# First two chunks of an mLSTM: exponents built on TensorE from the gate rows, and stabilizers, weights and states moved behind their outputs

## What is computed

```
for t in range(S):                       # every batch and head
    m_new  = max(f[t] + m, i[t])
    C = exp(f[t] + m - m_new) * C + exp(i[t] - m_new) * outer(v[t], k[t])
    n = exp(f[t] + m - m_new) * n + exp(i[t] - m_new) * k[t];  m = m_new
    y[t] = sigmoid(o[t]) * (C @ q[t]) / max(|n . q[t]|, 1)
x = y as (1536, 320);  h = x @ w_in      # 320 -> 2048
x = (h - tanh(h)) @ w_out                # 2048 -> 320
out = sum over 4 experts e of p[:, e] * (relu(x @ w1[e]) @ w2[e])   # 320 -> 1024 -> 320
```

## Time and profile before

| | |
|---|---|
| median of three runs | 649.0 us (648.75 to 649.26) |
| the profiled execution's own time | 649.84 us |
| its span in the trace | 648.0 us |
| TensorE (PE) busy | 96% of the span |
| DVE, ACT, POOL busy | 43%, 29%, 16% |
| first product of the layer-1 loop | at 42.75 us |
| mean DMA rate | 50 GB/s |

### The profile page before, as it was taken

How to read it: one execution, slowest core, us unless ns; L and a number is a source line. 1 busy time by engine, 2 the same in 40 slices (tenths; PEclk the granted TensorE clock), 3 DMA queues, 4 the chain that set the end, 5 groups by cost and what they waited for, 6 DMA issues and landing times.

```text
span 648.0 us, 8940 instructions
## 1 busy us (share of the span) xinstructions
PE 621.7 (96%) x3728; PEld 554.8 (86%) x3728; DVE 277.0 (43%) x504; ACT 185.7 (29%) x329; POOL 105.1 (16%) x87
## 2 busy tenths in 40 slices
PE   3997989999999999998999999999999999999998
PEld 2777988999878788887999999999999999999997
DVE  5576677776666465544131322313131331313132
ACT  2424534323442425455111232111321111111111
POOL 2356530000000000656000152000430000000000
PEclk8579799999999999999999999999999999999999
DMA  7254242112100000233100022000200000001011
GB/s 266 76 170 150 95 151 67 63 64 65 65 1 2 0 1 1 90 123 102 45 2 1 0 90 91 1 0 1 73 17 1 1 1 0 1 1 41 2 41 40
DMA packets 9831, 32.42 MB, mean 50 GB/s; under 512 B 1502, under 2 KB 3646, under 8 KB 9790
## 3 DMA queue, kind: packets, MB, share of 16 engines
q0 software_dynamic: 3456, 17.30, 7.8%
q1 hardware_dynamic: 6334, 14.54, 6.7%
HBM read 29.68 MB, written 1.97 MB: 49 GB/s over the span
## 4 chain that ended last, share of the span: by engine, by line
PE 84%; DVE 9%; ACT 3%; issue 2%; DMA 1%; SPq 0%; DVEq 0%; ACTq 0%
PE bank L858 9%; PE bank L859 9%; PE bank L860 9%; PE bank L900 9%; PE bank L901 9%; PE bank L902 9%; PE bank L862 5%; PE bank L861 5%; PE bank L877 3%; PE bank L762 3%; PE bank L878 3%; PE bank L879 3%; PE bank L753 2%; DVE g_lo L709 2%; DVE g_tmp L701 2%
## 5 line engine op out<-in xcount | busy, mean ns | idle before, releaser
L722 DVE SCALAR_TENSOR_TENSOR g_lo<-bank,g_hi 128x512 fp32r<-128x512 f32 x96 | 66.4, 692 | 256.3 <-ACT g_hi L514 256.2
L514 ACT ACTIVATE g_hi<-bank 128x512 fp32r<-128x512 f32 x96 | 57.5, 599 | 272.5 <-PE bank L862 272.4
L900 PE MATMUL bank<-w_all,g_hi 128*128 128x320 f32 x384 | 118.3, 308 | 1.5 <-DVE x_hi L679 1.5
L858 PE MATMUL bank<-x_hi,w_all 128*128 128x512 f32 (+2 forms) x320 | 118.9, 371 | 0.6 <-DVE x_hi L638 0.6
L859 PE MATMUL bank<-x_lo,w_all 128*128 128x512 f32 (+2 forms) x320 | 118.5, 370 | 0.0
L860 PE MATMUL bank<-x_hi,w_all 128*128 128x512 f32 (+2 forms) x320 | 118.3, 370 | 0.0
L901 PE MATMUL bank<-w_all,g_hi 128*128 128x320 f32 x384 | 118.3, 308 | 0.0
L902 PE MATMUL bank<-w_all,g_lo 128*128 128x320 f32 x384 | 118.2, 308 | 0.0
L386 POOL TENSOR_TENSOR w_all<-w_raw,w_all 128x1408 fp32r<-128x1408 f32 x16 | 51.4, 3211 | 238.6 <-ACT w_all L435 238.6
L900 PEld LDWEIGHTS bank<-w_all,g_hi 128*128 128x128 f32 x384 | 72.1, 188 | 5.5 <-issue 1.9
L901 PEld LDWEIGHTS bank<-w_all,g_hi 128*128 128x128 f32 x384 | 72.1, 188 | 4.5
(11 more groups left out here) (119 smaller groups left out, 741.2 us busy)
## 6 DMA issues: line engine op xcount, KB each, us to landing
w_raw<-in_w POOLq DMA_DIRECT2D x24, 704.0 KB, 4.4
feat<-in_feat SPq DMA_DIRECT2D x12, 512.0 KB, 4.1
tok<-in_tok SPq DMA_DIRECT2D x12, 484.0 KB, 5.6
out<-arena SPq DMA_DIRECT2D x12, 160.0 KB, 1.9
gst<-split SPq DMA_DIRECT2D x24, 4.0 KB
zx<-split SPq DMA_DIRECT2D x24, 4.0 KB
g_tmp<-in_gates SPq DMA_DIRECT2D x2, 48.0 KB
probs<-in_probs SPq DMA_DIRECT2D x1, 24.0 KB, 1.9
```

What stands on the lines that cost most here:

```text
L514: A(g_hi[:, b, 0:N], h_ps[b][:, 0:N], ACT.Relu).then_inc(ghi_ready, 1)
L722: V.scalar_tensor_tensor(g_lo[:, b, 0:N], h_ps[b][:, 0:N], 0.0, g_hi[:, b, 0:N].bitcast(F32), ALU.max, ALU.subtract).then_inc(g_ready, 1)
L858: mm(h, up_part(m, 0, k), x_hi[:, k, c], start=k == 0, stop=False)
L900: mm(out, g_hi[:, b, t], high_w, start=first, stop=False)
```

## The change

It has five parts. (1) Chunks 0 and 1 get their exponents without `gst` and `zx`: `first_exponents` multiplies `g_high` and `g_low` by columns of an identity `ident_r` spread over 512 columns, and for each head and each part of e one product of 128 columns with a broadcast identity column; then the mask. (2) The order on DVE is: gate rows, gate of chunk 0, scores of chunks 0 and 1, their rows (`first_rows`, read straight from the sums in PSUM), `x_low(0)`, then the stabilizers, `x_low(1)`, and the operand `zx`. The fillings of `gst`, `zx` and `state` go to POOL. (3) Weights (`wa`) and the states of chunks 0 and 1 stand inside the loop, at m = 0 and m = 1. (4) `START` of chunks 2 to 10 goes up by 4, 3, 2, 2, 2, 2, 1, 1 and 1; chunk 2 is wholly in the loop. Pieces 1 and 2 of the weights are split at the end of steps 0 and 1, and on POOL `split_low(0)` stands ahead of `weigh_v(0)`. (5) ACT's queue issues two of the three gate loads; SP's queue orders its loads as feat, tok of chunk 0, then of chunk 1, then of chunk 2 once tok of chunk 0 has landed, and its stacks begin with chunk 2.

```diff
-START = {2: -2, 3: 3, 4: 8, 5: 13, 6: 17, 7: 21, 8: 26, 9: 31, 10: 36, 11: 42}
+START = {2: 2, 3: 6, 4: 10, 5: 15, 6: 19, 7: 23, 8: 27, 9: 32, 10: 37, 11: 42}
-WARM_UP = 8
-FILL = 4
+WARM_UP = 3
-        split_at = {0: -1, 1: -1, 2: -1}
+        split_at = {0: -1, 1: 0, 2: 1}
...
+            for n in range(2):
+                load_feat(n)
+                load_tok(n)
+            sp.wait_ge(tok_in[0], 16)
+            load_feat(2)
+            load_tok(2)
+            sp.dma_start(probs[:, :, :], probs_d).then_inc(probs_in, 16)
...
+            stack(2)
+            stack(3)
             for n in range(RING, STEPS):
-                sp.wait_ge(e_ready, 2 * n - 2)
-                stack(n, z_high, z_low)
                 sp.wait_ge(sums_ready, n - RING + 1)
                 load_feat(n)
                 sp.wait_ge(y_ready, n - RING + 1)
                 load_tok(n)
+                if n + 1 < STEPS:
+                    sp.wait_ge(e_ready, 2 * n)
+                    stack(n + 1)
...
+            def first_rows(n, o_ps):
+                dve.wait_ge(intra_ready, n + 1)
+                after(dve, y_ready, n)
+                sums = heads(o_ps[:, 0:HEADS * HDE])
+                rows_out(n, sums[:, :, 0:HD], sums[:, :, HD:HDE].rearrange("p h a -> p (h a)"))
...
+            sigmoid(0)
             scores(0, 0, up_ps[0])
             scores(0, 1, up_ps[1])
-            sigmoid(0)
             scores(1, 0, bank[0])
             scores(1, 1, bank[1])
-            first_sums(0, c_ps, bank[4])
-            finish_rows(0)
+            first_rows(0, c_ps)
             sigmoid(1)
-            first_sums(1, up_ps[0], up_ps[1])
-            finish_rows(1)
+            first_rows(1, up_ps[0])
             x_low(0, c_ps)
+            stabilizers()
             x_low(1, up_ps[0])
...
+            def first_exponents(n, banks):
+                r = row0(n)
+                for q, out in enumerate(banks):
+                    picked = ident_r[:, r + q:r + HEADS:2]
+                    for k, rows in enumerate((g_high, g_low)):
+                        mm(out[:, :], rows, spread(picked, CH), start=k == 0, stop=False)
+                    for j in range(QUAD):
+                        row = r + 2 * j + q
+                        for rows in (e_high, e_low):
+                            mm(out[:, j * CH:(j + 1) * CH], ident_r[:, row:row + 1].to_broadcast([ROWS, P]), rows,
+                               start=False, stop=False)
+                    mm(out[:, :], ident_b[:, :], mask[:, :, :], start=False, stop=True).then_inc(e_ready, 1)
...
             for m in range(ALL_STEPS):
                 up(m)
+                if m == 0:
+                    weigh_columns()
+                if m == 1:
+                    new_state(0, a_ps, 0)
+                    new_state(1, b_ps, 0)
                 for n, k in phase(m):
                     attention(n, k)
```

More of the change, by code:

```diff
@@ L458, in _ @@
             A(e_high, er, ACT.Copy).then_inc(ehi_done, 1)
+            gate(0)
+            exps(0, 0, bank[0])
+            exps(0, 1, bank[1])
+            gate(1)
+            exps(1, 0, a_ps)
+            exps(1, 1, b_ps)
+            split_high(0)
+            x_high(0, c_ps)
+            x_high(1, up_ps[0])
             act.wait_ge(z_rows, 1)
@@ L465, in _ @@
             A(beta[:, :], decay[:, 0:ROWS], ACT.Exp).then_inc(beta_ready, 1)
[L466 to L481, removed]
             def evac(g):
@@ L516, in _ @@
                     evac(m // L1_TILES - 1)
-                for k in range(RING, PIECES):
+                for k in range(1, PIECES):
                     if split_at[k] == m:
@@ new lines, in rows_out @@
+            def rows_out(n, sums, nq):
+                chain.done(V.tensor_scalar(dn[:, :], nq, -1.0, None, ALU.mult))
+                chain.wait()
+                chain.done(V.scalar_tensor_tensor(dn[:, :], nq, 1.0, dn[:, :], ALU.max, ALU.max))
+                chain.wait()
+                chain.done(V.reciprocal(dn[:, :], dn[:, :]))
+                chain.wait()
+                o = tok[:, n % RING, 2 * D + HEADS:3 * D + HEADS].rearrange("p (h d) -> p h d", d=HD)
+                y = num[:, :, 0:HD]
+                chain.done(V.tensor_tensor(y, sums, spread(dn[:, :], HD), ALU.mult))
+                chain.wait()
+                after(dve, t_ready, n - 1)
+                V.tensor_tensor(yt[:, n % 2, :].rearrange("p (h d) -> p h d", d=HD), y, o, ALU.mult).then_inc(y_ready, 1)
@@ L794, in _ @@
                 mm(bank[7][:, 0:P], ident[:, :], ident[:, :], start=True, stop=True)
+            pe.wait_ge(identb_ready, 1)
+            pe.wait_ge(mask_ready, 1)
+            keep_warm(7, bank[7])
+            pe.wait_ge(identr_ready, 1)
+            pe.wait_ge(ghi_done, 1)
+            pe.wait_ge(glo_done, 1)
+            pe.wait_ge(ehi_done, 1)
+            pe.wait_ge(elo_done, 1)
+            first_exponents(0, bank[0:2])
+            scores(0, up_ps[0:2])
+            first_exponents(1, (a_ps, b_ps))
@@ L795, in _ @@
+            pe.wait_ge(exp_done, 2)
+            scores(1, bank[0:2])
+            keep_warm(3, bank[4])
+            intra(0, c_ps)
+            keep_warm(3, bank[4])
+            intra(1, up_ps[0])
             pe.wait_ge(top_ready, 1)
             for k, src in enumerate((top, cum)):
-                last = nc.tensor.transpose(c_ps[:, k * P:k * P + ROWS], src[:, CH - 1:CH].to_broadcast([ROWS, P]),
+                last = nc.tensor.transpose(bank[4][:, k * P:k * P + ROWS], src[:, CH - 1:CH].to_broadcast([ROWS, P]),
@@ L809, in _ @@
-            last.then_inc(weigh_t, 1)
-            pe.wait_ge(exp_done, 2)
-            scores(1, bank[0:2])
-            intra(0, c_ps)
-            pe.wait_ge(wa_ready, 1)
-            new_state(0, bank[4], 0)
-            pe.wait_ge(exp_done, 4)
-            both_exponents(2, (a_ps, b_ps))
-            intra(1, up_ps[0])
-            new_state(1, up_ps[1], 0)
-            pe.wait_ge(exp_done, 6)
-            scores(2, (a_ps, b_ps))
-            keep_warm(FILL, bank[0])
+            keep_warm(4, bank[3])
@@ L822, in _, with weigh_columns @@
             turn(0, c_ps)
-            keep_warm(FILL, bank[0])
+            keep_warm(8, bank[3])
             turn(1, up_ps[0])
-            keep_warm(FILL, bank[0])
+            keep_warm(6, bank[3])
+            def weigh_columns():
+                pe.wait_ge(weigh_done, 2)
+                pe.wait_ge(decay_ready, 1)
+                for k in range(2):
+                    last = nc.tensor.transpose(bank[4][:, k * ROWS:(k + 1) * ROWS], weigh[:, k, :],
+                                               ident[0:ROWS, 0:ROWS])
+                last.then_inc(weigh_t, 1)
```

149 lines of the change are left out of this document (61 added, 88 removed).

## The result

| | before | changed |
|---|---|---|
| median of four runs | 648.88 us (648.23 to 649.26) | 664.17 us (662.19 to 666.35) |
| the profiled execution's own time | 649.84 us | 666.35 us |
| its span | 648.0 us | 664.6 us |
| first product of the layer-1 loop | 42.75 us | 43.38 us |
| last product of up(16), start | 104.82 us | 111.87 us |

The ratio of the changed kernel to the one before is 1.0238, with a 95% interval of 1.0204 to 1.0271. The forecast was 648.0 us with a range of 642 to 652.5; the time lies outside it. Two of the ten runs of `a_gates_sp` (662.3 and 663.0 us) and, the other way, one of the six of `k_after_start9` (649.67 us) took some 12 us more or less than the rest of their kernel; none of the three has a trace, and the ratios compare the rest.

What follows compares the result with a forecast made beforehand. TensorE, busy 96% of the span, gains only where it waits or runs slowly: loop start 29.1 + 17.4 + 57.3 = 103.8 us to up(16) against 104.8, 1 us off the 649.0 median gives 648.0 us, range 642 to 652.5.

Steps and rivals of the forecast that it cites:

- Part 1, the clock: Ahead of the loop: clock rises about 1 us into the exponents, 0.4 us lost, bounds 0 and 6.4 us.
- The fifth rival: Half clock all the way ahead of the loop: loop starts at 40 us, time 659 us; chance 0.06.
- Part 1, the gates: At the start: two queues may bring gates up to 0.7 us sooner; counted as nothing, bounds 0 and 0.7 us.
- until about 7.1 us: Ahead of the exponents: seven keep_warm products at half clock, 0.43 us each, hold TensorE until then.
- Part 2: Steps 0 to 3: ACT waits for piece 3, so scores of chunk 2 start 17.4 us after the loop's start.
- Part 3: From the scores of chunk 2 to the last product of up(16): 57.3 us, against 46.8 us before.
- two more steps: Scores of chunk 2 to up(16): changed kernel has two extra steps, 1.95 us each with gaps, 3.9 us added.
- the comparison point: Start of the last product of up(16): 104.82 us before, forecast 103.8 us, 1 us faster.
- the later START: Behind up(16): START one or two steps later for chunks 5 to 10, counted 0, bound 0.5 us slower.
- 3.2 us by the prediction's count: Work moved into the loop: exponents and scores of chunk 2, states, weights; 3.2 us.

Runs made afterwards that it cites:

- a_gates_sp: Changed kernel with all three gate loads issued first on SP's queue, ahead of feat and tok, none by ACT: 650.92 us, ratio 1.0026.
- k_after_start9: Changed kernel with START of chunks 9 and 10 put back to 31 and 36, from 32 and 37: median 660.85 us.
- h_gates_warm2: Changed kernel with all gate loads first on SP's queue and 2 instead of 7 keep_warm products ahead of the exponents: 662.87 us, ratio 1.0216.
- b_warm14: Changed kernel with 14 instead of 7 keep_warm products ahead of the first exponents, gates still late: 651.62 us, ratio 1.0050.
- f_start9_back: Changed kernel with gates on SP, 9 keep_warm products, piece 3 split one step later, START of chunks 9 and 10 back: 648.6 us, ratio 0.9979.
- i_low_after_rows: Kernel before with first_exponents for chunks 0 and 1, 9 keep_warm, and POOL's low parts held until the rows stand: 640.37 us, ratio 0.9854.
- j_low_and_fill: As i_low_after_rows, with eight instead of four unread wide products ahead of each of the two transposes of rows: 640.19 us, ratio 0.9859.
- e_before_filled: Kernel before with 28 more keep_warm products while TensorE waited for zx: 646.9 us, ratio 0.9965.

## Why the prediction was wrong

**Part 1, the clock, failed, and with it the forecast.** The text took "a rise about 1 us into the exponents (0.4 us lost)" with "bounds 0 and the full 6.4 us". In the changed kernel the clock rose at 41 us, 30 us after the exponents had begun. The bound was too narrow as well, since it let only the exponents be slow: scores, fillings and intra behind them were slow too. The reason given was that TensorE runs wide products "without a gap" from about 4 us on. There was a gap of 2.37 us ahead of the exponents. `h_gates_warm2` and `b_warm14` show from both sides that the clock decides: same gates with less filling 662.87 us, late gates with more filling 651.62. From the first exponents to the loop's start it took 33.0 us where the sum had 22.0, so this term was off by 11.0 us: 12.1 by the clock (`a_gates_sp` takes 20.9 us for the same stretch, 7.33 to 28.26), less 1.1 by which the sum was too long. The fifth rival named this outcome with a loop start at 40 us and 659 us, and gave it 0.06.

**Part 1, the gates, failed.** They were counted at "0 and 0.7 us" earlier and came 3 us later; the exponents began at 10.38 instead of 7.1 us, off by 3.3 us. Two of three gate loads stand on ACT's queue, the last asked for at 2.44 us, and had to share the engines with the loads of feat and tok that SP asked for from 1.75 us on; the last gate landed 5.55 us after its issue. In the kernel before the last was asked for no earlier, at 2.60 us, but ahead of feat and tok, and DVE used it at 5.03. With all three ahead of feat and tok on SP's queue the scan starts at 4.96 us. The Trainium skill, "DMA: Bandwidth & Descriptors", section "Issuing engines are not separate DMA queues", also says that transfers interleave on the same engines whoever starts them. The trace agrees; I had used only its half on issue time, and not asked what interleaves with the gates. The gap behind the filling comes from this delay, so the two failures are one chain. The filling itself came later too, at 4.84 us against 3.72 in `a_gates_sp`: ACT makes `ident_b`, for which it waits, only after it has issued the two loads. The prediction had it run "until about 7.1 us"; it ended at 8.01. That the filling would have been too short even with the gates in time is ruled out by `a_gates_sp`, which reached its loop at 28.26 us against the 29.1 that I had forecast for the changed kernel.

**Part 2 was right.** 18.35 us measured, 17.4 forecast, by the same chain and with the same wait on ACT. The load of piece 3 took 6.8 us to ACT's start where I had 5.5.

**Part 3 was 2.8 us too long.** From the scores of chunk 2 to up(16) it took 50.1 us; the scores and sums of chunk 5, which my 57.3 included and which now stand behind up(16), add 4.3, so 54.5 us. Of the 2.8 us, 1.95 are a step too many: the sum took "two more steps", but the scores of chunk 2 stand at step 3 in the changed kernel and those of chunk 3 at step 4 before, which is one more. The windows confirm half clock in 61.7 to 68 us, 6.3 us at 0.51 and so about 3.1 us lost, where I had kept 3.4.

**Behind the comparison point the later START was counted at "0 (bound 0.5 us slower)"; 5.2 us were lost there.** From up(16) to the end it is 552.7 us, of which 4.3 are the work of chunk 5 named above, against 543.2 before. I had seen that the rows of chunk 8 come at step 31, and not that the exps of chunk 9 then meet the evaluation of group 2's inputs at step 32. `k_after_start9` gives 3.6 us back; where the other 1.6 are lost is not shown.

**The terms add up.** 14.3 (gates 3.3, clock 11.0) + 0.95 - 2.8 + 5.2 = 17.6 us; the forecast span was 647.0, the measured one 664.6, that of the slowest of the four runs.

**Where did the 14 us of the early start go in `a_gates_sp`?** The structure of the forecast holds there: its loop is 14.5 us earlier and its time the same as before. Part 2's wait on ACT is in its trace too (8.07 us before L435 at 42.74), and the scores of chunk 2 start 18.15 us after the loop. That its traced span is 647.0 us, the very number of the forecast, is in part luck: with the 4.3 us of chunk 5 it is 2.1 us ahead of the forecast at up(16) (97.42 us), and the same 2.1 us are lost behind it, where the forecast had 0; its median is 650.92. The rest is lost at steps 0 to 16, seen best between two kernels without the loss at step 34. From the loop's start to up(16), with the sums of chunk 5 in it, `f_start9_back` takes 72.5 us (28.32 to 96.46, and 4.3), `i_low_after_rows` 64.0 (30.33 to 94.36), and the kernel before 62.1. The work that the change moves into the loop is 3.2 us by the prediction's count. The other 5 us are waits and half clock: from its loop's start to 60 us TensorE is idle for 6.7 us at a mean clock of 0.78 in `f_start9_back`, and for 4.1 us at 0.84 in `i_low_after_rows`. So the new exponents were the gain, and moving weights, states and chunk 2 behind the loop's start, which was to clear the way to it, gave back more than the 2 us of earlier start that it brought over `i_low_after_rows`. How much each of these moves gave back alone is not separated.

## What to carry to other kernels

When a forecast rests on the clock, look for the idle time directly ahead of the dense work and at what ends it. Filling products must reach up to that work, sized by the latest plausible arrival of what it waits for; too many cost nothing that could be measured (`b_warm14`, `j_low_and_fill`), too few cost 12 us here. And small transfers that everything waits for belong in front of the large ones in time of issue; a second issuing engine did not put them there.

## What the runs showed of the hardware

- One filling of seven wide products, followed by idle times of 0.41, 1.69 and 2.37 us, left the exponents at full clock, at full clock for one bank and then at half, and at half from the start. In the changed kernel TensorE then worked from 10.4 to 41 us nearly without idle time at the durations of half clock, on products of 512, 128 and 41 columns; what it did just before the rise was eight `keep_warm` products between two sets of transposes; in the kernel before it was four.
- The Trainium skill, "TensorE: Matmul & The Clock Gate", section "HAM oscillation — how this bites in real kernels", describes work that begins at the low clock after each wait; its waits are of 3 to 5 us. The traces agree for the waits of 2.37 and 2.83 us ahead of the exponents and in part for that of 1.69 us (the second bank), not for those of 0.41, 0.69 and 1.43 us (`e_before_filled`). In the loop the same wait goes both ways: behind 1.50 us ahead of the sums of chunk 3 the clock fell in `i_low_after_rows` (0.52 from 54 to 60 us) and stayed at 1.00 in `j_low_and_fill`. Nor does a fall need a wait: ahead of the loop of `i_low_after_rows` the clock was at half from about 23.5 to 27 us, and TensorE had not been idle for more than 0.22 us at a time since 8 us. What decides between such cases is not shown here.

```profile
23.00:24.00 1.00, 1.00 (x17) 0.78 (x14) 0.97 (x2) 0.00 (x0) 0.97 (x1) 0.74 0.27 23
24.00:25.00 1.00, 1.00 (x5) 0.40 (x4) 1.00 (x1) 0.00 (x0) 1.00 (x2) 0.50 0.67 163
```

- Eight products of 128 columns with a weight load each take 1.80 us at half clock and 1.00 at full. Two banks of four heads took 3.2 us at full clock (7.33 to 10.51), as the 1.6 us per bank of the forecast had it.
- DVE's product of two operands in SBUF waited 3.4 us for POOL's three operations, while the other engines' work went on. The Trainium skill, "SBUF — State Buffer", section "SBUF: two separate sides", calls the port pair that DVE and GpSimd share an exclusive lock, held for a whole instruction, for DVE operations with two SBUF inputs too. The trace agrees on the kind of operation; here DVE got it only after three instructions of POOL in a row, and moving those freed it. That is one case: in the same trace `g_lo` (L710), also with two operands in SBUF, took its usual 0.43 us at 46.60, where one instruction of POOL ends and the next begins. And a `TENSOR_SCALAR` with one such operand took 1.44 us beside POOL (L587 at 35.81) against 0.31 (at 26.81).
